# Fetching a tile's rows at their full pitch of 768 bytes in place of 528

## The reference, cut to what matters

```
kv_flat = kv.reshape(B, H//4, 4, W//4, 4, C).mean(axis=(2, 4)).reshape(B, -1, C) @ w_sr
k = v = kv_flat                                    # 768 keys a batch
x = softmax(q @ k.T / sqrt(C)) @ v                 # 24576 rows of 128

# layer 1, 8 experts, F = 1024
e = argmax(x @ w_gate);  g = softmax(x @ w_gate)[e]
x = g * (relu(x @ w1[e]) @ w2[e])

# layer 2 is the same with one more factor, the opened gate of the row's expert
x = g * sigmoid(x @ w_output_gate)[e] * (relu(x @ w1[e]) @ w2[e])
```

## Time and profile before

| | |
|---|---|
| Median of three runs | 1875.98 us (1874.28 to 1877.02) |
| Profiled execution, first to last instruction (span) | 2009.7 us |
| Mean granted TensorE clock in it | 0.986 |
| PE busy | 1918.1 us, 95% of the span |
| DVE, ACT, POOL busy | 67%, 52%, 37% |
| HBM read and written | 98.41 MB and 87.63 MB |

### The profile page before, as it was taken

The page is one execution under the profiler, slowest core; times in us unless marked ns, Lnnn a source line. Parts: engine busy times, 40 slices in busy tenths (PEclk is TensorE's granted clock), DMA queues, the critical chain, the costliest instruction groups (busy, mean ns, idle before and its releaser), DMA issues. The chain is left out here.

```text
span 2009.7 us, 53289 instructions
## 1 busy us (share of the span) xinstructions
PE 1918.1 (95%) x15716; PEld 1879.5 (94%) x15716; DVE 1342.6 (67%) x3525; ACT 1054.8 (52%) x2333; POOL 739.4 (37%) x823
## 2 busy tenths in 40 slices
PE   9999999999999999998999989899999999999998
PEld 7999999999999989898898889888999999999998
DVE  6788887888887666565566666666655555555555
ACT  3777777777776344344344444343444444444444
POOL 5456643466643323222222222222333333333333
PEclk8999999999999999999999999999999999999999
DMA  8355532355533211111321111142211114141111
GB/s 301 104 169 174 178 102 74 109 172 175 173 114 125 67 49 50 42 46 44 118 92 44 45 48 42 51 135 74 66 44 46 43 42 165 42 163 43 46 44 36
DMA packets 138040, 185.88 MB, mean 92 GB/s; under 512 B 17425, under 2 KB 95380, under 8 KB 134368
## 3 DMA queue, kind: packets, MB, share of 16 engines
q1 hardware_dynamic: 112640, 134.16, 20.9%
q0 software_dynamic: 25312, 50.65, 7.1%
HBM read 98.41 MB, written 87.63 MB: 93 GB/s over the span
## 5 line engine op out<-in xcount | busy, mean ns | idle before, releaser
L1718 DVE SCALAR_TENSOR_TENSOR h_lo<-psum,h_hi 128x512 fp32r<-128x512 f32 x800 | 541.2, 688 | 248.3 <-ACT h_hi L1509 198.4
L1509 ACT ACTIVATE h_hi<-psum 128x512 fp32r<-128x512 f32 x800 | 460.6, 598 | 259.1 <-PE psum L1303 244.9
L1303 PE MATMUL psum<-x_hi,w 128*128 128x256 f32 x1600 | 344.7, 290 | 66.6 <-DVE x_lo L1712 48.7
L413 POOL DMA_INDIRECT y_bucket<-kv_store,place x200 | 194.3, 971 | 542.1 <-DVE place L379 484.5
L1303 PE MATMUL psum<-x_hi,w_split 128*128 128x256 f32 x1600 | 339.6, 287 | 9.2 <-issue 2.8
L997 POOL DMA_INDIRECT out<-rows x200 | 193.9, 970 | 405.0 <-DVE rows L1738 368.5
L1303 PEld LDWEIGHTS psum<-x_hi,w 128*128 128x128 f32 x1600 | 270.2, 192 | 75.5 <-issue 55.2
L1320 PE MATMUL psum<-h_hi,w 128*128 128x256 f32 x1600 | 321.6, 285 | 0.7 <-DVE h_lo L1718 0.7
L413 POOL DMA_INDIRECT x_bucket<-rows,place x192 | 190.0, 990 | 293.2 <-DVE place L379 197.7
L1303 PEld LDWEIGHTS psum<-x_hi,w_split 128*128 128x128 f32 x1600 | 265.5, 189 | 17.4 <-issue 10.5
L1320 PEld LDWEIGHTS psum<-h_hi,w 128*128 128x128 f32 x1600 | 266.4, 195 | 1.3 <-DVE h_lo L1718 1.3
(11 more groups left out here) (177 smaller groups left out, 4385.1 us busy)
## 6 DMA issues: line engine op xcount, KB each, us to landing
w_table<-w_split SPq DMA_DIRECT2D x64, 512.0 KB, 3.5
w_raw<-in_moe_w SPq DMA_DIRECT2D x64, 256.0 KB, 4.1
xr<-x_bucket SPq DMA_DIRECT2D x100, 132.0 KB
xr<-y_bucket SPq DMA_DIRECT2D x100, 132.0 KB
kv_store<-in_kv SPq DMA_DIRECT2D x24, 512.0 KB, 9.3
q_in<-in_q SPq DMA_DIRECT2D x48, 256.0 KB, 2.7
w<-w_table SPq DMA_DIRECT2D x12, 1024.0 KB, 6.8
w_split<-w_table SPq DMA_DIRECT2D x8, 1024.0 KB
```

Source lines behind the costliest of these rows:

```text
L413: nc.gpsimd.indirect_dma_start(r.bucket[:, :], bass.IndirectOffsetOnAxis(r.place[:, g, s:s + 1], 0), r.rows[:, g, s, LG:], None, bounds_ch ...
L1303: ins = nc.tensor.matmul(bank[p][:, m * BLOCK:(m + 1) * BLOCK], layer.w1[c % 2][:, hl, f], x[:, c % 2, :], start=k == 0, stop=k == 2)
L1509: nc.scalar.activation(h_hi[:, p, :], bank[p][:, :], ACT.Relu).then_inc(h_hi_done, 1)
L1718: nc.vector.scalar_tensor_tensor(h_lo[:, p, :], bank[p][:, :], 0.0, h_hi[:, p, :].bitcast(F32), ALU.max, ALU.subtract).then_inc(h_lo_done, 1)
```

## The change

`PITCH` becomes 192, the whole line. The fetch then takes 384 floats into a slot of 384 floats, so a partition's part is one run of 1536 bytes on both sides. The same holds for the writes of `neutral` (L563 and L910), and `neutral` itself grows from 264 to 384 floats per partition. All tensors that are allocated behind `neutral` move up by 480 bytes; `pad_xr` grows by 8 floats, so that `xr` moves by 512 bytes. What is scattered is as before.

```
-PITCH = 132
+PITCH = 192
 LINE = 192
...
-        sb("pad_xr", [P, 40])
+        sb("pad_xr", [P, 48])
         xr_slots = sb("xr", [P, 4, 384])
         xr = xr_slots[:, :, 0:SUB * PITCH].rearrange("p k (s c) -> p k s c", c=PITCH)
```

## The result

The changed kernel takes 1880.63 us (1880.19 to 1884.96, seven runs) against 1874.77 us for the kernel before (1872.91 to 1877.02, seven runs). The ratio is 1.0033, with a 95% interval of 1.0023 to 1.0043: 0.33% slower, or some 6 us. The forecast was "no change", 1876 us; the time lies in the range of 1868 to 1882, but the change is slower by more than the 0.2% that I had called no change, and the time is just outside the 1872 to 1880 that I gave the forecast itself. The range holds it by its margin and not by its reasons.

The account below looks back on a forecast made before the run. PE was taken to bound the kernel, busy 1918.1 of 2009.7 us; every term of the change was 0 us on the path, so 2009.7 + 0, less 133.7 us to the runs' median, gave 1876.0 us, range 1868 to 1882.

Parts of the forecast that it names:

- Bound and path: PE bounds the kernel; the fetch into `xr` is on no visible path, some 16 us of slack against about 2.
- the sum: Profiled execution 2009.7 us plus 0 for the change; the runs' median is 133.7 us lower, giving 1876.0 us.
- The data: A fetch grows from 135.2 to 196.6 KB, +0.04 us of DMA time, 8 us over 200 fetches, all hidden.
- The bounds from windows: Fetch cost bounded by rates of neighbouring transfers in the trace: between 0.04 us less and 0.08 us more.
- The issue: SP issues a fetch in 338 ns in place of 553, about 0.2 us a tile, with time in plenty: 0 us.
- Reading `xr`: PE's transposes load a slot's second half from byte 768 in place of 528; the odd start costs nothing: 0 us.
- `neutral`: Its fill on POOL at the start grows by 0.10 us, within slack; its 16 later writes are far ahead: 0 us.
- The moved tensors: The rest that moves by 480 bytes is small tensors: 0 us.
- The slow one: Layer 1: scatters land 0.3 us later, VectorE loses 15 us, about half reaches PE: 1883 us, chance 0.16.
- The fast one: Layer 1: fewer runs shorten PE's `x_lo` stalls: 1869 us, or 1860 if the clock doesn't fall; chance 0.20.
- The signs: If right: L752 about 340 ns, HBM reads about 110.7 MB, no PE wait ending with `xr`, layer 1 `x_lo` stalls unchanged.
- The two times: The profiled execution's 2009.7 us and the runs' median 133.7 us lower; the profiled execution was taken to be slower.

Follow-up runs that it names:

- experiment 4: The changed kernel with the fetch alone undone, again two runs of 528 bytes for each partition: 1881.41 us, ratio 1.0031 to the kernel before.
- experiment 12: The changed kernel with the token's number and gate in columns 136 and 137, on the chip where the kernel before takes 2010.26 us: 2000.41 us, ratio 0.9936.
- experiment 5: The kernel before with only the second row of an `xr` slot moved, to byte 768 in place of 528: 1880.72 us, ratio 1.0028.
- experiment 7: The changed kernel with `xr` moved 32 bytes further (`pad_xr` 56 in place of 48): 1876.43 us, ratio 1.0004 to the kernel before.

## Why the prediction was right or wrong, point by point

**Bound and path: right on the usual chips.** PE bounds the kernel, the fetch is off the path. Undoing the fetch alone changes nothing (experiment 4). But the sum began from the 2009.7 us of the other condition, "2009.7 + 0", and for that one the 0 doesn't hold: the kernel nearest to the change (experiment 12) took 0.6% less there.

**The data: wrong in size, without effect.** I took +0.04 us a fetch, at most +0.08. From the share of q1, 22.6% of 1872.6 us before on a usual chip and 24.4% of 1878.8 us after, the 16 engines are busy for 423.2 and 458.4 us; that is 35.2 us over 216 transfers of this form (200 fetches, 16 of `neutral`), +0.16 us each on about 0.51. The bounds from windows were too narrow, since a window's rate holds what else moves in it. The estimate from the Trainium skill ("DMA: Bandwidth & Descriptors", section "How a descriptor splits into AXI transactions"), +27% or 0.14 us, was the nearer one. A fetch still lands sooner, 2.4 us in the median after its issue where it was 2.6; the issue itself is 0.2 us shorter.

**The issue: right.** 337 ns on SP in place of 553, and SP went on waiting:

```profile
L752 SPq DMA_DIRECT2D xr<-x_bucket x100: 331/337/358, 616.2 to 1254.0; - x100
```

**Reading `xr`: this step failed.** I put it at 0 us: "the odd start costs nothing that going away could give back", from the durations of the loads themselves. That sentence holds, but it asks only about the old places, and the new ones are the bad ones. The durations of the loads held no answer, 139 to 153 ns before and 138 to 156 after, since the cost falls on the matmuls behind them, some 4.5 ns on each in one tile of four. It is some 5 of the 6 us: experiment 5 has it alone (1.0028), experiment 7 takes it away (1.0004).

**`neutral`: right as far as could be measured. The moved tensors: put at 0, and they cost about 0.9 us.** Experiment 7 still has both and is within 0.13% of before, but the attention is longer in each kernel where the small tensors moved, 25.11 us against 25.07 for four blocks. Which of the tensors does it wasn't tried.

**The rivals.** The slow one, by the scatters, named a wait that did grow, from 8.4 to 12.7 us, with the long fetch and not with the places: 12.0 to 12.9 us in the four kernels on the usual chips that have the long fetch and 7.4 to 8.5 in the five that don't. Experiment 7 has the wait without the loss and experiment 4 the loss without the wait, so it is covered. The fast one is seen on the slow chip alone. The time came out slower for a cause that none of my rivals held; that it is as near to 1876 as it is owes something to the step being small.

**The signs.** L752 took 337 ns, 110.70 MB were read from HBM, and no wait of PE ended with `xr`, as forecast. "As many and as long" stalls of `x_lo` held on the slow chip; on the usual chips there are none in either kernel.

**The two times.** I read 133.7 us between the span and the median as the cost of profiling and went on. They were two conditions, and the stalls, the falls of the clock and the idle time of layer 1 that the first part speaks of belong to one of them.

## What to carry to other kernels

When an edit changes the stride or the base of anything that TensorE reads, treat the new addresses as a change of its own: put the padding back so that the starts fall where they were, or try two or three of them, before judging the rest of the edit. When all waits are the same and a PE-bound loop still takes longer, compare the time between the same instruction in two rounds of the loop; a step of 0.2 us in 23.6 shows there and in no busy share. Then go one level down, from tile to tile and from matmul to matmul: an average of 1 ns a matmul was in truth some 4.5 ns in one tile of four. And when a profiled span and the median of the runs differ by more than a percent or two, find out first whether they are of the same chip and condition.

## What the runs showed of the hardware that I had not expected

PE's stream of matmuls of 256 columns has two paces at the same granted clock, 113.4 and 118 ns from start to start, and a tile keeps the slow one until the next transposes. Two 128x128 fp32 blocks, loaded by PE once a tile, bring one tile in four of layer 2 into the slow pace at one pair of start addresses, and not at the five other pairs tried, in which one or both lie 16 to 80 bytes further; that is 0.2 us in 23.6. Layer 1, with the same loads and the matmuls of L1335 in place of the transposes of L1337, has 3 to 5 slow tiles in every kernel on the usual chips. The same program took 1875 us on two chips and 2010 us on another, in all 21 runs there; ScalarE got the transposed rows up to 3.37 us after their start in place of 0.42 (medians by place in the body). And one edit had opposite signs on the two: slower by 0.3% on the one, and faster by 0.6 to 0.8% in the three kernels nearest to it on the other.
